# Order of work in the first batch, the wait for the bias, and who splits the spatial weights, in a scan, rotation and gated-MLP kernel

## The reference

```
state = alpha_t * state + k_t v_t^T ;  x_t = q_t state          # per head, 768 steps
theta = x @ w_theta ;  z = (x cos(theta), x sin(theta))
u = x + w_tok_r @ z_cos + w_tok_i @ z_sin                       # mixes tokens
x2 = u + relu(u @ w_ch)
h = relu(x2 @ w_in) ; gate, v = halves of h (512 wide each)
v = (v - mean) / sqrt(var + 1e-6)                               # per token
out = (gate * (w_spatial @ v + b_spatial)) @ w_out
```

## Time and profile before

| | |
|---|---|
| median of 3 runs | 617.14 us (615.31 to 619.04) |
| the profiled execution | 616.59 us |
| its span, from first to last instruction | 614.90 us |
| TensorE busy | 586.9 us, 95% |
| VectorE, ScalarE, GpSimd busy | 364.6, 223.4, 260.4 us |
| mean granted TensorE clock | 0.994 of full |

### The profile page before, as it was taken

One profiled execution on the slowest core, in us unless ns is written; L12 is line 12 of the kernel. 1 busy time (PEld: TensorE's weight loads), 2 busy tenths in 40 slices (PEclk: granted clock), 3 DMA queues, 4 the chain that ended last, 5 costly groups with the idle time before them and its releaser, 6 DMA issues.

```text
span 614.9 us, 11189 instructions
## 1 busy us (share of the span) xinstructions
PE 586.9 (95%) x4608; PEld 556.3 (90%) x4608; DVE 364.6 (59%) x564; ACT 223.4 (36%) x411; POOL 260.4 (42%) x208
## 2 busy tenths in 40 slices
PE   3898898999999999999999999899999999999998
PEld 3687788999999999999999989898999899989997
DVE  5799688687667876877643347537233723372132
ACT  2555454443353433433443216414131323142110
POOL 5656397554353434643513036636113611362130
PEclk9999999999999999999999999799999999999999
DMA  8652111133131311421123190200220020002002
GB/s 315 219 202 102 65 65 66 66 111 122 48 121 66 104 65 66 150 80 57 51 103 116 46 341 1 77 1 2 77 78 2 1 78 1 1 0 78 0 2 78
DMA packets 20259, 49.54 MB, mean 81 GB/s; under 512 B 1648, under 2 KB 15216, under 8 KB 19696
## 3 DMA queue, kind: packets, MB, share of 16 engines
q1 hardware_dynamic: 20208, 48.81, 22.8%
HBM read 39.37 MB, written 9.44 MB: 79 GB/s over the span
## 4 chain that ended last, share of the span: by engine, by line
PE 79%; DVE 8%; ACT 4%; POOL 3%; issue 2%; DMA 2%; SPq 0%; DVEq 0%; ACTq 0%; POOLq 0%
PE psY L413 20%; PE psY L532 6%; PE psC L445 6%; PE psC L395 5%; PE psS L532 4%; PE psF L532 4%; PE psY L506 4%; PE psS L346 3%; PE psF L374 3%; PE psC L532 2%; PE psY L516 2%; PE psS L506 2%; PE psF L496 2%; DVE akq L780 2%; DVE after L771 2%
## 5 line engine op out<-in xcount | busy, mean ns | idle before, releaser
L986 POOL TENSOR_TENSOR z_lo<-cos_sin,z_hi 128x768 fp32r<-128x768 f32 x23 | 43.0, 1869 | 107.6 <-ACT z_hi L627 107.5
L1056 POOL TENSOR_TENSOR gated_lo<-u_gated,gated_hi 128x384 fp32r<-128x384 f32 x32 | 32.4, 1012 | 126.7 <-ACT gated_hi L731 126.6
L780 DVE TENSOR_TENSOR_SCAN akq<-akq,rtotal 128x516 f32<-128x516 f32 x24 | 57.1, 2381 | 0.9
L413 PE MATMUL psY<-tok_r_hi,z_hi 128*128 128x384 f32 x141 | 51.1, 362 | 2.1 <-POOL tok_i_lo L980 1.5
L969 POOL TENSOR_TENSOR akq<-akq,after 128x512 f32<-128x512 f32 x24 | 44.4, 1848 | 9.0 <-DVE after L771 7.4
L413 PE MATMUL psY<-tok_i_lo,z_hi 128*128 128x384 f32 x141 | 47.3, 335 | 0.0
L413 PE MATMUL psY<-tok_i_hi,z_lo 128*128 128x384 f32 x141 | 47.3, 335 | 0.0
L413 PE MATMUL psY<-tok_r_hi,z_lo 128*128 128x384 f32 x141 | 47.2, 335 | 0.0
L413 PE MATMUL psY<-tok_i_hi,z_hi 128*128 128x384 f32 x141 | 47.2, 335 | 0.0
L413 PE MATMUL psY<-tok_r_lo,z_hi 128*128 128x384 f32 x141 | 47.1, 334 | 0.0
L731 ACT ACTIVATE gated_hi<-u_gated 128x384 fp32r<-128x384 f32 x32 | 16.8, 525 | 82.5 <-DVE u_gated L920 82.5
(11 more groups left out here) (222 smaller groups left out, 1753.3 us busy)
## 6 DMA issues: line engine op xcount, KB each, us to landing
akq<-akq SPq DMA_DIRECT2D x23, 770.0 KB, 4.4
v<-v_in SPq DMA_DIRECT2D x24, 192.0 KB, 4.8
x_dram<-u_f SPq DMA_DIRECT2D x8, 576.0 KB, 3.7
x_raw<-x_dram SPq DMA_DIRECT2D x4, 1152.0 KB, 5.2
out<-ot SPq DMA_DIRECT2D x24, 192.0 KB, 1.9
raw_tok_r<-w_tok_rT SPq DMA_DIRECT2D x6, 384.0 KB, 7.7
raw_tok_i<-w_tok_iT SPq DMA_DIRECT2D x6, 384.0 KB, 8.9
raw_sp<-w_spT SPq DMA_DIRECT2D x1, 2304.0 KB, 9.2
```

Of the source, the lines that this page charges most:

```text
L413: mm = pe.matmul(psY[:, j, 0:HALF], Z[s][l][:, q, tile(j)], W[m][:, s, half(h)], start=(s == 0 and q == 0 and n == 0), stop=(s == CHUNKS - ...
L780: dve.tensor_tensor_scan(ALPHA[s], ALPHA[s], rtotal[:, 1:], rtotal[:, 0:1], ALU.mult, ALU.add).then_inc(decayed, 1)
L986: pool.tensor_tensor(Z[c][1][:], trigs[g % 2][:], f(Z[c][0][:]), ALU.subtract).then_inc(z_lo, 1)
L1056: pool.tensor_tensor(GA[1][:, j, half(h)], ug[h][:, j], f(GA[0][:, j, half(h)]), ALU.subtract).then_inc(g_lo, 1)
```

## The change

It has three parts. In the first batch TensorE does one third of a token unit, then x's transposition, then the other two thirds; ScalarE makes the high part of the transposed x ahead of the sines and its copy ahead of z's high part; VectorE makes the low part of the transposed x ahead of the product with sine and cosine. The last six pieces of the token weights are split one chunk earlier each, and w_ch is split ahead of them. In the second stage the wait for the bias stands at the first gate and not ahead of the first moments, the first two moments and the first `norm` stand ahead of the last three `make_x2`, and VectorE makes all six low parts of the spatial weights.

```diff
-SPLITS = ((0, 1), (2,), (3,), (4,), (5,), (), (6, 7), (8, 9), (10, 11)) + ((),) * (BATCH * CHUNKS)
+SPLITS = ((0, 1), (2,), (3,), (4,), (5,), (6, 7), (8, 9), (10, 11)) + ((),) * (BATCH * CHUNKS)
...
@@ TensorE, first batch
-                token_mix(FIRST_UNITS[c])
+                token_mix(FIRST_UNITS[c], (0,))
                 transpose_x(c)
+                token_mix(FIRST_UNITS[c], (1, 2))
@@ TensorE, spatial_mix
-                        if s < SP_VECTOR:
-                            pe.wait_ge(sp_lo, s + 1)
-                        else:
-                            pe.wait_ge(sp_lo_end, s + 1 - SP_VECTOR)
+                        pe.wait_ge(sp_lo, s + 1)
@@ ScalarE, first batch
                 for i in SPLITS[c]:
                     tok_high(i)
+                xT_high(c)
                 if c:
                     sines(c - 1)
-                xT_high(c)
+                keep_xT(c)
                 if c:
                     z_high(c - 1)
-                keep_xT(c)
@@ ScalarE, later batches
-                    for i in SPLITS[g]:
-                        tok_high(i)
                     if g == CHUNKS:
                         act.wait_ge(ch_in, 16)
                         act.activation(WC[0][:], raw_ch[:], ACT.Copy).then_inc(ch_hi, 1)
+                    for i in SPLITS[g]:
+                        tok_high(i)
@@ VectorE, first batch
                 update_state(c)
+                xT_low(c)
                 if c:
                     multiply_z(c - 1)
-                xT_low(c)
@@ VectorE, gate
                 dve.wait_ge(gi_relu, n + 1)
+                if n == 0:
+                    dve.wait_ge(bias_in, 16)
@@ VectorE, second stage
             make_u(HALVES * b + 1)
+            find_moments(0, 0)
+            find_moments(0, 1)
+            norm(0, 0)
             for m in range(CT):
                 make_x2((HALVES * b + 1) * CT + m, last_banks[m])
 
-            dve.wait_ge(bias_in, 16)
...
-                    for c in range(SP_VECTOR):
+                    for c in range(CHUNKS):
                         dve.wait_ge(sp_hi, c + 1)
                         dve.tensor_tensor(WS[1][:, c, :], raw_sp[:, c, :], f(WS[0][:, c, :]),
                                           ALU.subtract).then_inc(sp_lo, 1)
@@ GpSimd, later batches
-                    for i in SPLITS[g]:
-                        tok_low(i)
                     if g == CHUNKS:
                         pool.wait_ge(ch_hi, 1)
                         pool.tensor_tensor(WC[1][:], raw_ch[:], f(WC[0][:]), ALU.subtract).then_inc(ch_lo, 1)
+                    for i in SPLITS[g]:
+                        tok_low(i)
@@ GpSimd, second stage
-                    for c in range(SP_VECTOR, CHUNKS):
-                        pool.wait_ge(sp_hi, c + 1)
-                        pool.tensor_tensor(WS[1][:, c, :], raw_sp[:, c, :], f(WS[0][:, c, :]),
-                                           ALU.subtract).then_inc(sp_lo_end, 1)
```

More of the change, by code:

```diff
@@ L41 @@
 VSLOTS = 3
-SP_VECTOR = 4
 SEG = P + 1
@@ L203, in build @@
         in_in, sp_in, out_in, bias_in = sems("in_in sp_in out_in bias_in")
-        in_hi, in_lo, sp_hi, sp_lo, sp_lo_end, out_hi, out_lo = sems("in_hi in_lo sp_hi sp_lo sp_lo_end out_hi out_lo")
+        in_hi, in_lo, sp_hi, sp_lo, out_hi, out_lo = sems("in_hi in_lo sp_hi sp_lo out_hi out_lo")
         x2_in, x2_hi, x2_lo = sems("x2_in x2_hi x2_lo")
@@ L937, in _ @@
             make_u(HALVES * b + 1)
+            find_moments(0, 0)
+            find_moments(0, 1)
+            norm(0, 0)
             for m in range(CT):
                 make_x2((HALVES * b + 1) * CT + m, last_banks[m])
-            dve.wait_ge(bias_in, 16)
             for b in range(BATCH):
-                find_moments(b, 0)
-                for i in range(1, CHUNKS):
+                if b:
+                    find_moments(b, 0)
+                for i in range(1 if b else 2, CHUNKS):
                     find_moments(b, i)
```

## The result

| | |
|---|---|
| changed kernel, median of 19 | 613.38 us (611.47 to 615.04) |
| kernel before, median of 19, same runs | 616.69 us (615.31 to 619.04) |
| ratio | 0.9948 (0.9936 to 0.996) |
| profiled execution, its span | 615.04 us, 613.3 us |

The kernel is 3.3 us faster where 7.4 was forecast, and 613.38 lies outside the range of 607.0 to 613.0. Three points of the timeline split the profiled execution. The first `channel_mix` starts at 98.01 us, 4.65 later than before (93.36). The first spatial product starts at 386.10, 4.85 later than in the earlier trace rows. The next product starts 6.24 us behind it, where it took 12.65: 6.41 won. So 4.85 - 6.41 = -1.56, which is 613.3 - 614.9 but for rounding. In this execution the second stage gave all that was forecast, and the first batch took most of it back.

A forecast was written before the change was run, and what follows sets the result against it. TensorE is busy 95% of the span, so only its waits and half-clock time can be won. 614.9 - 6.4 (spatial weights) - 1.0 (first batch) = 607.5 us span, given as 609.5 measured against 617.14; range 607.0 to 613.0.

The forecast's parts named there:

- The second stage: Spatial weights: high parts come 3.2 us earlier, no low part is late, stops and half clock go; -6.4 us.
- Steps 1 and 2: First batch: xT_low ahead of the product makes the period 10.68 us; chunk 5's angles start at 68.85, 1.4 us earlier.
- step 3: Chunk 5: two token-weight pieces go ahead of chunk 4's z_lo; TensorE's next unit starts at 74.4, 0.8 us later.
- Step 5: Before channel_mix: u_lo ends at 93.4, +0.1 us (range 92.9 to 94.9); the later token-weight wait goes, 1.27 us won.
- the clock falls in the first batch instead: Rival: two close TensorE stops of 1.7 and 2.2 us bring half clock, +3 us, 612.5; chance 0.17.
- the slower case: Rival: TensorE, waiting longer for VectorE each first-batch chunk, loses its clock for long; some 620 us; chance 0.02.
- the first batch's worst end: First batch: both token-weight pieces slip ahead of the product in chunk 5; +1.0 us at worst.

The follow-up runs named there:

- e1: Kernel before with only the second-stage part: bias wait and first moments moved, all six spatial low parts on VectorE; 610.46 us, ratio 0.9912.
- e4: Kernel before with only the token-weight splits one chunk earlier and w_ch split ahead of them; 617.92 us, ratio 1.0039.
- e2: Kernel before with only the first-batch part: thirds, new orders, earlier splits, w_ch first; 619.19 us, ratio 1.0051.
- e3: Kernel before with only the first batch's thirds and new orders on ScalarE and VectorE, splits as before; 615.62 us, ratio 0.9987.
- g1: Changed kernel with w_ch split behind the two pieces of token weights again; 608.63 us, ratio 0.9884.
- f1: e1 plus token-weight splits one chunk earlier, w_ch left behind the pieces; 609.81 us, ratio 0.99.
- f4: Kernel before with only all six spatial low parts on VectorE, bias wait left in place; 612.61 us, ratio 0.9945.
- g4: Kernel before with only the bias wait and first moments moved, GpSimd keeping two spatial low parts; 611.11 us, ratio 0.9925.

## Why the prediction was right in one part and wrong in the other

**The second stage: right.** Every step is in the trace: moments released by v, `relu_v` 3.1 us earlier (3.2 forecast), the last low part 0.95 us early (1 forecast), no stop, the clock full, -6.41 for -6.4. Its size holds for the profiled execution. By medians it is -5.6 (e1). Four profiles have the old second stage, and they take 12.65 (the kernel before), 11.64 (e4), 11.42 (e2) and 9.55 us (e3) from the first product to the next, at a granted clock of 0.73, 0.85, 0.85 and 1.00. e3 has the same stops for GpSimd's pieces (1.26 and 1.02 us) and no half clock. So the gain is 3.3 to 6.4 us by execution, and the forecast took its top from one profile.

**Steps 1 and 2: right but for the tie.** The period is 10.67, and `angles` of chunk 5 starts at 68.86 in g1, 68.81 in e2 (68.85 forecast); in the profiled execution of the changed kernel it is 71.70, by the tie of step 3.

**Step 3: right where the tie falls as assumed.** The unit starts at 74.40 and 74.45 in e2 and g1 (74.4). In the profiled execution of the changed kernel GpSimd's piece and the angles' last instruction came at once and GpSimd had it, which put z_lo of chunk 4 at 74.66, 2.16 us behind g1's. I gave a margin of 0.1 us for another tie, the product's, and took this one from a row of chunk 4 without asking what happens if it is lost.

**Step 5: the step that failed.** "The same work in another order", with "I take 93.4, +0.1" for u_lo's end. The late end that I worked out, 94.9, is what the chip does: u_lo ends at 94.64 in e4, which has the splits and w_ch first alone. I had both ends and the mechanism, and took the mild one without following VectorE's instructions through the new order under the lock as I had stated it. The term went in at +0.1 us, with +1.5 as its late end, and no half clock behind either. In median, w_ch's place costs 4.75 us (g1 against the changed kernel). In profiles, e4 against f1, it is 3.0: `channel_mix` 1.5 us later and 1.5 us of half clock behind it. Without any half clock it is 3.0 in the new order (the executions at 1.000 under g1). The other 1.7 of the median can be the half clock at `channel_mix`, the half clock in the last chunk as in e2, or the lost tie as in the profiled execution; their shares, and what makes the tie fall one way or the other, are open.

**The rival that came true in part** is "the clock falls in the first batch instead", at 0.17. Its price, 612.5, is near the 613.38, but that is partly luck: most of the loss is the late u_lo, which the rival did not have. The clock fell behind its two stops in e2 and not in g1 (1.60 and 2.20 us, full clock). And it fell behind a stop not named, the single one of 2.9 us at `channel_mix`, in all three profiles with w_ch first (0.77 from 96.58 to 104.00 in e2, 0.73 from 94.74 to 101.00 in e4), though not in the two executions of the changed kernel at 1.000. What I held against it, one stop of 2.95 us that left its slice at 9, was one execution: f1, f4 and e4 have the same stop at full clock too, and g4 has it with 0.50 behind it. I should have given the case more, and tied it to step 5's late end, since a late u_lo is such a stop. The longest dip that cost time is g4's 6.0 us at 0.50, 3.0 lost, and the slower case did not come.

The range failed by 0.4 us because the first batch's worst end (+1.0) had neither u_lo's late end together with the loss of step 3 nor any half clock in it; by medians the first batch costs 3.2 us (e2) where -1.0 was forecast. The sum itself has a slip of 0.2: 609.2 + 0.5 is 609.7 and not 609.5, which changes nothing here. The forecast is near what the change gives with w_ch left in its place (608.63).

## What to carry to other kernels

Where two engines exclude each other, "the same work in another order" isn't free: write out both engines' instructions through the new order, with who holds the lock, before taking it at nothing. A long instruction that another engine must wait out can be a shield for what comes behind it. When an end of a bound makes TensorE stop for about 3 us, add the half clock behind it to that bound (1.5 us here). And look where the engine that waits sits: half clock costs time only where TensorE sets the pace.

## What the runs showed of the hardware

- VectorE's scans, products and the angles' last instruction take turns with GpSimd's, instruction by instruction, and each waits out the other's. The scan takes 1.23 us alone, 1.43 behind half a z_lo, 2.25 behind a whole one. The angles' last instruction (fp32, one SBUF input) takes 2.02 and 1.97 us for 0.36. The low part of the transposed x, with an input in PSUM, does not wait: 0.55 us at 71.10 in the changed kernel, inside a GpSimd piece that runs from 70.92 to 72.86.
- The Trainium skill (GPSIMD Engine Reference, "Specifications") names contention for VectorE instructions in a 2-port perf mode or with two SBUF inputs. The trace agrees for the scan, which has two; which mode the angles' last instruction ran in, no view here shows.
- The same stop does not always cost the clock. 2.95 and 2.94 us ahead of `angles` gave 1.00 in one execution and 0.50 in another; the stops for sp_lo gave 0.50 in the kernel before and 1.00 in e3. One execution's clock row therefore does not say what the next one will do.
- Half clock is not always lost time. In e1 the granted clock is 0.58 from 25.0 to 31.5 us and 0.57 from 60 to 64, while VectorE sets the pace, and the first `channel_mix` still starts at 93.17, for 93.36 in the kernel before.
